# Sliding-window attention on one NeuronCore: sink columns in plain fp32, and the scores of two heads in the two row halves of TensorE

## The reference, cut to what matters

```
scores = scale * np.matmul(q, k.transpose(0, 1, 3, 2))
is_sink = pos[None, :] < int(n_sink)
in_window = (rel >= 0) & (rel < int(window))
scores = np.where(is_sink | in_window, scores, -1000000000.0)
a = np.exp(scores - np.max(scores, axis=-1, keepdims=True))
a = a / (np.sum(a, axis=-1, keepdims=True) + 1e-09)
attn = np.matmul(a, v)                      # (2, 8, 768, 64) -> x (1536, 512)
h = x @ w_in;  x = (h * np.tanh(softplus(h))) @ w_out
out = sum_e p[:, e:e + 1] * (np.maximum(x @ w1[e], 0.0) @ w2[e])     # 4 experts
```

## Time and profile before

| | |
|---|---|
| time, median of 3 runs | 958.93 us |
| the 3 runs | 959.03, 958.93, 956.46 us |
| span of the profiled execution | 956.4 us |
| PE, PEld busy | 906.0 us (95%), 732.4 us (77%) |
| DVE, ACT, POOL busy | 463.7, 311.1, 265.3 us |
| first score matmul | 7.07 us |
| first score of rounds 1, 2 and 3 | 36.87, 70.20 and 101.30 us |
| last score, first matmul of the feed-forward layers | 131.33, 140.8 us |

### The profile page before, as it was taken

The page is one execution under the profiler, slowest core; times in us unless marked ns, Lnnn a source line. Parts: engine busy times, 40 slices in busy tenths (PEclk is TensorE's granted clock), DMA queues, the critical chain, the costliest instruction groups (busy, mean ns, idle before and its releaser), DMA issues.

```text
span 956.4 us, 12645 instructions
## 1 busy us (share of the span) xinstructions
PE 906.0 (95%) x4240; PEld 732.4 (77%) x4240; DVE 463.7 (48%) x915; ACT 311.1 (33%) x605; POOL 265.3 (28%) x234
## 2 busy tenths in 40 slices
PE   5788888999996999999999999999999999999998
PEld 4566566778884888777888888888888888888887
DVE  7888877887789888884121221212121211212121
ACT  4666654454444545453111231111311112211110
POOL 4644434522255325287200240000330002400000
PEclk9999989999997999999999999999999999999999
DMA  7122311100022000013000130000320001001011
GB/s 227 53 79 79 112 46 48 45 0 2 0 66 86 24 0 0 0 66 110 1 1 0 44 109 22 0 0 0 109 67 0 0 0 63 25 0 44 0 44 44
DMA packets 14847, 38.66 MB, mean 40 GB/s; under 512 B 3296, under 2 KB 4064, under 8 KB 14816
## 3 DMA queue, kind: packets, MB, share of 16 engines
q1 hardware_dynamic: 14656, 37.91, 12.5%
q10 hardware_dynamic: 160, 0.39, 0.2%
HBM read 35.15 MB, written 3.15 MB: 40 GB/s over the span
## 4 chain that ended last, share of the span: by engine, by line
PE 71%; DVE 16%; ACT 7%; issue 5%; POOL 1%; DMA 1%; DVEq 0%; ACTq 0%
PE banks L588 33%; PE banks L441 33%; DVE pool L1008 5%; DVE pool L1005 2%; PE banks L466 2%; DVE pool L1002 2%; ACT pool L735 2%; DVE pool L1014 2%; ACT pool L738 2%; ACT g_hi L720 1%; ACT pool L638 1%; DVE w_hi L916 1%; PE banks L525 1%; DVE pool L874 1%; DVE w_hi L923 1%
## 5 line engine op out<-in xcount | busy, mean ns | idle before, releaser
L1058 DVE SCALAR_TENSOR_TENSOR g_lo<-banks,g_hi 128x512 fp32r<-128x512 f32 x96 | 66.2, 691 | 393.0 <-ACT g_hi L749 393.0
L441 PE MATMUL banks<-x_hi,w_hi 128*128 (+1 forms) x576 | 224.9, 390 | 0.0
L441 PE MATMUL banks<-x_lo,w_hi 128*128 (+1 forms) x576 | 224.6, 390 | 0.0
L441 PE MATMUL banks<-x_hi,w_lo 128*128 (+1 forms) x576 | 224.3, 389 | 0.0
L336 POOL TENSOR_TENSOR w_lo<-w_raw,w_hi 128x1024 fp32r<-128x1024 f32 (+1 forms) x52 | 119.8, 2306 | 343.2 <-ACT w_hi L712 343.2
L749 ACT ACTIVATE g_hi<-banks 128x512 fp32r<-128x512 f32 x96 | 57.4, 598 | 422.7 <-PE banks L441 422.7
L588 PE MATMUL banks<-w_hi,g_hi 128*128 128x512 f32 x384 | 149.4, 389 | 0.0
L588 PE MATMUL banks<-w_lo,g_hi 128*128 128x512 f32 x384 | 149.4, 389 | 0.0
L588 PE MATMUL banks<-w_hi,g_lo 128*128 128x512 f32 x384 | 149.4, 389 | 0.0
L441 PEld LDWEIGHTS banks<-x_hi,w_hi 128*128 128x128 f32 x576 | 108.8, 189 | 22.6
L441 PEld LDWEIGHTS banks<-x_hi,w_lo 128*128 128x128 f32 x576 | 108.4, 188 | 22.8
(11 more groups left out here) (73 smaller groups left out, 993.3 us busy)
## 6 DMA issues: line engine op xcount, KB each, us to landing
w_raw<-weights SPq DMA_DIRECT2D x48, 512.0 KB, 3.4
pool<-kT SPq DMA_DIRECT2D x8, 400.0 KB, 3.8
pool<-v SPq DMA_DIRECT2D x8, 384.0 KB, 3.2
out<-pool SPq DMA_DIRECT2D x12, 256.0 KB, 2.1
pool<-qT SPq DMA_DIRECT2D x14, 192.0 KB, 3.2
pool<-qT ACTq DMA_DIRECT2D x2, 192.0 KB, 5.0
pool<-vs SPq DMA_DIRECT2D x8, 48.0 KB, 2.7
p_raw<-probs SPq DMA_DIRECT2D x1, 24.0 KB, 7.7
```

Source lines behind the costliest of these rows:

```text
L441: mm = pe.matmul(banks[:, 4 + f % H_RING, :], w[:, f, k * P:(k + 1) * P], x[:, k, ds(c * CHUNK, CHUNK)], start=(k == 0 and n == 0), stop=( ...
L1058: dve.scalar_tensor_tensor(out=g_lo[:, f % G_RING, :], in0=banks[:, 4 + f % H_RING, :], scalar=0.0, in1=g_hi[:, f % G_RING, :].bitcast(f32 ...
```

## The change

- `q_pad` (2 batches x 2 heads x 768 columns, half of it zeros) becomes `q_pair` (2 x 768, both heads, no zeros). The memsets of the zeros go, and each q load is one DMA of 128 rows instead of two of 64.
- The score matmul of a head takes only its own 64 rows of `q_pair` and `k_pair`. The scores of units i and i+1 are issued together, at the even stage, before turn(i-7).
- `stack_sinks` and `split_values` go. GpSimd multiplies all 272 columns. TensorE transposes the 16 sink columns of each head by itself (two transposes for one), VectorE copies 16 x 256 instead of 96 x 128, and the sinks' part of the output is two plain fp32 matmuls of 128 rows and 64 columns with `v_sink`, which holds the 16 sink values and zeros below. A memset at the start makes the zeros.
- The tiles lie elsewhere in `pool`.

```
         Q_AT = 0
-        K_AT = Q_AT + B * 2 * S
+        K_AT = Q_AT + B * S
         V_AT = K_AT + B * KW
-        SCORES_AT = V_AT + B * QT * P
+        SINKS_AT = V_AT + B * QT * P
+        SINK_T_AT = SINKS_AT + B * P
+        SCORES_AT = max(SINK_T_AT + 4 * 2 * P, NC * CT * CHUNK)
...
                 if part == "q":
-                    for hd in range(2):
-                        rows = slice(D * hd, D * hd + D)
-                        sp.dma_start(q_pad[rows, b, hd, :], qT[b, ds(ct, 1), rows, :].rearrange("a p n -> (a p) n"))\
-                            .then_inc(qk_in[b], 16)
+                    sp.dma_start(q_pair[:, b, :], qT[b, ds(ct, 1), :, :].rearrange("a p n -> (a p) n"))\
+                        .then_inc(qk_in[b], 16)
...
-                    if not isinstance(ct, int) or b > 0:
-                        sp.wait_ge(v_stack_done, ct * (2 * B) + 2 * b)
-                    sp.dma_start(v_stack_raw, vs[b, ds(ct, 1), :, :].rearrange("a p n -> (a p) n"))\
-                        .then_inc(v_stack_in, 16)
+                    if isinstance(ct, int) and b == 0:
+                        sp.wait_ge(sink_zero, 1)
+                    sp.dma_start(v_sink[0:SINKS, b, :], vs[b, ds(ct, 1), :, :].rearrange("a p n -> (a p) n"))\
+                        .then_inc(v_in[b], 16)
...
-            pl.wait_ge(ident_done, 2)
-            pl.memset(q_pad[D:P, 1, 0, :], 0.0).then_inc(pad_zero[1], 1)
-            pl.wait_ge(pad_zero[1], 1)
-            pl.memset(q_pad[0:D, 1, 1, :], 0.0).then_inc(pad_zero[1], 1)
...
-                    if windowed and j >= 2 and j % 2:
-                        p = p[:, SINKS:]
-                    if windowed and j >= 2 and j % 2 == 0:
-                        p = prob_of[windowed][:, u % ring, 0:2 * (P + SINKS)]\
-                            .rearrange("p (a n) -> p a n", a=2)[:, :, 0:P]
...
                     for key, col, n in segments[j]:
-                        mm = pe.matmul(s_bank[windowed][u % SCORE_BANKS[windowed]][:, col:col + n], q_pad[:, b, hd, j * P:(j + 1) * P],
-                                       k_pair[:, b, key:key + n], start=True, stop=True)
+                        rows = slice(D * hd, D * hd + D)
+                        mm = pe.matmul(s_bank[windowed][u % SCORE_BANKS[windowed]][:, col:col + n], q_pair[rows, b, j * P:(j + 1) * P],
+                                       k_pair[rows, b, key:key + n], start=True, stop=True)
...
-                            pe.wait_ge(stacked, ct * STACKS + done + 1)
...
-                            mm = pe.transpose(banks[0:6 * SINKS, SINK_BANK, 0:P],
-                                              stack[:, done % 4, :, :, :].rearrange("p k h n -> p (k h n)").bitcast(f32),
-                                              ident[:, :])
+                            first = 0 if j % 2 else P
+                            for h in range(2):
+                                mm = pe.transpose(banks[0:SINKS, SINK_BANK, P * h:P * h + P],
+                                                  prob_of[True][:, (u - 1 + h) % PROB_RING[True], first:first + SINKS],
+                                                  ident[:, :])
...
-                        mm = pe.matmul(banks[:, out_bank, column], v_stack[:, b, :], stack_T[:, done % 4, :],
-                                       start=False, stop=True, skip_group_check=True)
+                        for h in range(2):
+                            mm = pe.matmul(banks[D * h:D * h + D, out_bank, column], v_sink[:, b, D * h:D * h + D],
+                                           sink_T[:, done % 4, h, :], start=False, stop=True, skip_group_check=True)
...
                 def stages(ct, i, before):
-                    if i < UNITS:
-                        score(ct, i)
+                    if i < UNITS and i % together == 0:
+                        for u in range(i, i + together):
+                            score(ct, u)
...
-            act.dma_start(q_pad[0:D, 0, 0, :], qT[0, 0, 0:D, :]).then_inc(qk_in[0], 16)
-            act.dma_start(q_pad[D:P, 0, 1, :], qT[0, 0, D:P, :]).then_inc(qk_in[0], 16)
+            act.dma_start(q_pair[:, 0, :], qT[0, 0, :, :]).then_inc(qk_in[0], 16)
...
+            dve.memset(part(SINKS_AT, B * P + 4 * 2 * P), 0.0).then_inc(sink_zero, 1)
...
-            dve.memset(q_pad[D:P, 0, 0, :], 0.0).then_inc(pad_zero[0], 1)
-            dve.memset(q_pad[0:D, 0, 1, :], 0.0).then_inc(pad_zero[0], 1)
...
-                        dve.tensor_copy(stack_T[:, done % 4, :], banks[0:6 * SINKS, SINK_BANK, 0:P])\
+                        if early(ct, u, 6):
+                            dve.wait_ge(sink_zero, 1)
...
+                        dve.tensor_copy(sink_T[0:SINKS, done % 4, :, :].rearrange("p h n -> p (h n)"),
+                                        banks[0:SINKS, SINK_BANK, 0:2 * P])\
...
-                    for n in range(2):
-                        at = unit_at(ct, i, INVERT_LAG[windowed] + n, before)
-                        if windowed and at and at[1] % together == 0 and (at[1] // 2 + n) % QT >= 2:
-                            stack_sinks(at[0], at[1] + 2 * n)
-                    if i < UNITS and i % (UNITS // B) == SPLIT_VALUES_AT:
-                        split_values(ct, i)
```

More of the change, by code:

```diff
@@ L134, in part @@
             return t
-        q_pad = part(Q_AT, B, 2, S)
+        q_pair = part(Q_AT, B, S)
         k_pair = part(K_AT, B, KW)
@@ L144, in build @@
         prob_T = part(TURNED_AT, 4, 512)
-        v_stack_raw = part(SINKS_AT, 1, P)[0:6 * SINKS, 0, :]
+        v_sink = part(SINKS_AT, B, P)
+        sink_T = part(SINK_T_AT, 4, 2, P)
         acc = part(0, NC, CT, CHUNK)
@@ L200, in build @@
         mask_ready = sem("mask_ready")
-        pad_zero = [sem(f"pad_zero{b}") for b in range(B)]
+        sink_zero = sem("sink_zero")
         full_iota = sem("full_iota")
@@ L213, in build @@
         turned_out = sem("turned_out")
[L214 to L217, removed]
         sink_out = sem("sink_out")
@@ L455, in attention @@
                 groups = 1 if windowed else 2
+                together = 2 if windowed else 1
                 def score(ct, u):
@@ L459, in score @@
                     if u % (2 * QT) == 0:
-                        pe.wait_ge(qk_in[b], 48 * ct + 48)
+                        pe.wait_ge(qk_in[b], 32 * ct + 32)
                     if not early(ct, u, SCORE_BANKS[windowed]):
@@ L505, in pv @@
                     if j == 0 and units[0] % 2 == 0:
-                        pe.wait_ge(v_in[b], 16 * ct + 16)
+                        pe.wait_ge(v_in[b], 32 * ct + 32)
                     if j % 4 == 0 and units[0] % 2 == 0:
@@ L562, in _ @@
             pe.wait_ge(flag_ready, 1)
-            pe.wait_ge(pad_zero[0], 2)
-            pe.wait_ge(pad_zero[1], 2)
+            pe.wait_ge(sink_zero, 1)
             small = pe.value_load(flag[0:1, 0:1])
@@ L905, in stack_sinks @@
-                def stack_sinks(ct, u):
-                    j, slot = u // 2 % QT, stacks_before(u) % 4
-                    dve.wait_ge(den_ready, ct * (UNITS // together) + u // together + 1)
-                    if not early(ct, u, 8):
-                        dve.wait_ge(turned, ct * UNITS + u - 6)
-                    first = 0 if j % 2 else P
-                    at = ct * (2 * STACKS) + 2 * stacks_before(u)
-                    for h in range(2):
-                        p = prob_of[True][:, (u + h) % PROB_RING[True], first:first + SINKS]
-                        dve.tensor_scalar(stack[:, slot, 0::2, h, :],
-                                          p.rearrange("p (a n) -> p a n", a=1).to_broadcast([P, 2, SINKS]),
-                                          row_den[:, (u + h) % 8:(u + h) % 8 + 1], None, ALU.mult)\
-                           .then_inc(stack_step, 1)
-                    for h in range(2):
-                        p = prob_of[True][:, (u + h) % PROB_RING[True], first:first + SINKS]
-                        dve.wait_ge(stack_step, at + h + 1)
-                        low = dve.scalar_tensor_tensor(out=stack[:, slot, 1, h, :], in0=p,
-                                                       scalar=row_den[:, (u + h) % 8:(u + h) % 8 + 1],
-                                                       in1=stack[:, slot, 0, h, :].bitcast(f32),
-                                                       op0=ALU.mult, op1=ALU.subtract)
-                        if h:
-                            low.then_inc(stacked, 1)
@@ L1099 @@
     vt = np.ascontiguousarray(v.reshape(B, CT, 2, QT, P, D).transpose(0, 1, 4, 3, 2, 5)).reshape(B, CT, P, QT, P)
-    v_sinks = np.zeros((B, CT, 3, 2, SINKS, 2, D), v.dtype)
-    for h in range(2):
-        v_sinks[:, :, :, h, :, h, :] = v.reshape(B, CT, 2, S, D)[:, :, None, h, 0:SINKS, :]
-    v_sinks = v_sinks.reshape(B, CT, 6 * SINKS, P)
+    v_sinks = np.ascontiguousarray(vt[:, :, 0:SINKS, 0, :])
     up1 = moe_w_in.reshape(CT, P, F1 // P, P).transpose(2, 1, 0, 3).reshape(F1 // P, P, CT * P)
```

21 lines of the change are left out of this document (1 added, 20 removed).

## The result

The changed kernel took 933.0 us (median of four runs: 931.53, 932.76, 933.24, 934.57) against 958.71 for the kernel before (four runs, 956.46 to 959.03). The ratio is 0.9736, with a 95% interval of 0.9720 to 0.9752.

A forecast was written before the change was run, and what follows sets the result against it. VectorE, whose masks stand behind the sink stack, was taken as the bound. Savings of 7.6 (rounds 1 to 3), 2.3 (round 0), 1.2 (way out) and 0.1 (start) sum to 11.2 us: span 945.2, forecast 948, range 938 to 965.

The forecast's parts named there:

- rivals 1 and 2: Score halves side by side only in part, 955 us, chance 0.17; one after the other, 963 us, chance 0.12.
- The loop between the engines: A pair's second score waits for the previous pair's first mask: 2.2 to 2.4 us, below TensorE's 2.48.
- 31.1 less 4.6 of waits is 26.5 of work: Round 2: its time less TensorE's waits for masks and ScalarE's copy, taken as TensorE's work before the change.
- plus 0.8: TensorE's work per round rises by 0.8 us with the change, giving 27.3 us in round 2.
- The 0.14 for each pair's 16-column transposes: Sink transposes on TensorE: a layout change of their own, 0.14 us per pair, bounds 0 and 0.14.
- Of the waits I leave the 1.2 for ScalarE's copy: Round 2: TensorE's 1.2 us wait for ScalarE's copy stays after the change, making the round 28.5 us.
- I keep 2.9 for drops: Rounds 1 and 3: one clock drop each, about 2.2 and 0.7 us, kept after the change.
- rival 3: Attention: more drops of the granted clock; eight more use up the gain, sixteen give 972 us; chance 0.11.
- can't fall much below 27.5: Round 0: GpSimd needs 23.3 us and starts late, so 29.8 us falls to 27.5, saving 2.3 us.
- Way out: End of attention: two pairs' stacks, 3.0 us, go; ScalarE and TensorE hide part, so 1.2 us is saved.
- Start: Before the first score: fewer q loads and a changed memset save 0 to 0.5 us, taken as 0.1.
- Rival 4: Better: sink transposes on the whole array, waits of 0.6 us per round, 941.5 us; chance 0.20.

The follow-up runs named there:

- no_stack: The kernel before without the four stack instructions per pair on VectorE, so the sinks' part of the output is missing: 928.3 us.
- first_whole: The changed kernel with the scores of the first six pairs as whole-array matmuls on zero-padded q, the rest in halves: 928.78 us.
- sinks_only: The kernel before with only the new handling of the sinks; whole-array scores on q_pad, one unit per stage: 933.88 us.
- reorder_first_whole: first_whole with products with v right behind the scores and both units' transposes together: 924.5 us.
- halves_only: The kernel before with q_pair, scores of 64 rows and two units at a time; the stack stays on VectorE: 972.92 us.
- halves_apart: The changed kernel with each head's 64-row score alone at its own stage: 1034.27 us median, four runs between 999.77 and 1051.44.

## Why the prediction came out as it did

**Right.** VectorE's stack, slow beside GpSimd, set the pace: put back alone it takes back the gain, taken away alone (`no_stack`) it brings 30 us. The halves run side by side, which refutes rivals 1 and 2. TensorE's pair was 2.42 us where I summed 2.48; the four score records took 0.66, a little over my 0.5 to 0.6. The loop between the engines, which I had put at 2.2 to 2.4 us, took 2.1 (scores at 63.37, the mask ends at 65.49). The rule that matmuls start in program order (the Trainium skill, TensorE: Matmul & The Clock Gate, Part 3), which I had read record by record, gave three steps for the scores. For records the trace speaks against it here too: there are two steps, with the records of a step 7 ns apart. Taken for whole matmuls, nothing here contradicts it. The feed-forward layers stayed within 3 us; their 1.2 lies within what they differ by in the kernels here, 813.0 to 815.5 us with the same instructions.

**Wrong: "31.1 less 4.6 of waits is 26.5 of work".** `no_stack` measures 25.5. An idle time begins in the trace at the end of a record, and the next record could have started earlier: two scores start 0.46 us apart, and a pair of them ends 0.62 after its start. So a round less its idle time comes out above the work, by an estimated 0.16 us for each of the six waits in the round, 1.0 in all. I had also subtracted 0.40 us too many, which hid part of this: one of the five waits of the earlier trace rows for the masks ends at 70.20 us, ahead of the round, and without it the difference is 27.0, which is TensorE's busy time in the earlier trace rows. So the method is off by 1.4, and my figure by 1.0. My own steps said it: 8 x 2.36 with sinks, 2 x 2.03 for j = 1 (scores of 0.87, no sinks) and 2 x about 1.2 for j = 0 are an estimated 25.3; I built the sum on the difference instead.

**Wrong: "plus 0.8".** It was 0.4. The 0.14 for each pair's 16-column transposes did not exist (8 x 0.14 = 1.1 us), while the layout changes around the scores cost more than I had for them (0.81 us for the scores with them, not 0.74; 0.19 into the row halves and 0.15 out, not 0.28).

**Wrong: "Of the waits I leave the 1.2 for ScalarE's copy".** None was left in round 2, nor in that of `no_stack`: with masks on time ScalarE is on time too. 1.2 us per round. The three terms, 1.0, 0.4 and 1.2, make the 2.6 us of round 2's error (28.5 against 25.9). Over rounds 1 to 3 the errors are 2.4, 2.6 and 2.9, 7.9 in all; 1.1 of the last is the line between rounds and way out.

**Wrong: "I keep 2.9 for drops".** The granted clock did not fall in attention. The drops followed waits (the first, at 56.9 us, came behind waits of 1.03 and 0.58 us from 53.5 on), and I had named that against rival 3, but not used it in the forecast. With 7.9 this gives the 10.8 us by which rounds 1 to 3 came out better.

**Round 0: "can't fall much below 27.5".** It took 25.4, and in `no_stack` and `first_whole` 23.4 and 23.05. I had given GpSimd 23.3 us of work in it, and the earlier trace rows already had its busy time there as 18.0: two of the eight weight pieces (37.0 and 42.6 us) and four of the 24 multiplications lie behind the round. After, it is 16.2, and GpSimd does not bound the round. The half-speed clock, which I had not foreseen, costs 2.3 us (25.4 against `first_whole`).

**Way out: 3.3 us and not 1.2.** The other engines hid little of the last stacks, and the drop of the clock that followed them went too. The kernel before, timeline of TensorE:

```profile
138.90 0.42 PE L495 MATMUL banks<-ident,w_hi 128*96 128x128 f32 x1 [1.61 <-DVE w_hi L934]
139.25 1.12 PE L525 MATMUL banks<-pool 128*64 128x128 f32 x8
```

One wait of 1.61 us for VectorE, and eight records behind it in 1.12 us where 0.66 is their length at full clock.

**Start: 0.5 us later and not 0.1 earlier.** It is the one term that went the other way, by 0.6. The q load in one DMA of 128 rows goes with it: the nine kernels that have it start their scores at 7.38 to 7.56 us, the five with two of 64 rows (before, `sinks_only`, `no_stack`, `first_whole`, `reorder_first_whole`) at 6.97 to 7.10, some of these with the long memset of zeros. The traces show what is late. VectorE works on the parameters from 5.1 to 5.3 us on instead of 3.9 to 4.0, when their load has landed, and the last load that the first score waits for is that of the keys, not that of q. Why the one DMA does this was not tried.

All these errors but that of the start point one way, so the range of 938 to 965 could not cover them: I had let each doubtful term stand at its dear end, and called that the likeliest value.

**Rival 4** had the right direction and still left waits and drops. **Rival 3**, the clock, showed in `halves_only` and `halves_apart`, in the two runs with the stack's work put back and, small, in round 0: the range was right to reach to it.

## What to carry to other kernels

When a wait between engines goes, don't subtract the idle times of the trace: add up the starts of the waiting engine's own work, piece by piece, and take that as the new time. Judge a small instruction by where it stands, not by its engine's mean load: four short operations per pair, right behind the instruction that releases GpSimd, cost over 5 us in a round of 26. Half-size matmuls pay where they stand in pairs with few changes of layout between them, and can lose more than that where TensorE waits or its clock is not up yet.

## What the runs showed of the hardware that was not expected

- Two 16-column operations of VectorE in SBUF took 1.22 us beside GpSimd's multiplications and 0.37 us after them. The masking, from PSUM, was not slowed: in the change, 272 wide, it takes 439 ns in the mean beside them and 428 away from them.
- Two fp32 matmuls in different row halves start together although the second has a wait of its own: four records of 272 columns in 0.66 us. Going into the row halves costs 0.19 us, out of them 0.15.
- With scores in halves TensorE stayed at half speed until 22.3 us in the change and until 206.4 us when each stood alone, and fell to it for 44 us in `halves_only`. Whole-array scores in the first six pairs brought full speed at 12.9 us.
